# xLSTM block with two feed-forward layers in one kernel: layer one in four chunks of 2, 3, 3 and 4 tiles

## What is computed

```python
for t in range(S):                       # B, H = 2, 8; S = 768; D = 40
    m_new = np.maximum(f_gate[t] + m, i_gate[t])
    f_stab, i_stab = np.exp(f_gate[t] + m - m_new), np.exp(i_gate[t] - m_new)
    C = f_stab * C + i_stab * outer(v[t], k[t]);  n = f_stab * n + i_stab * k[t]
    y[t] = sigmoid(o_gate[t]) * (C @ q[t]) / np.maximum(np.abs(n @ q[t]), 1.0)
x = y.reshape(1536, 320)
xn = x / rms(x) * rms_g                  # layer one, 1536 hidden features
x = (silu(xn @ w_gate) * (xn @ w_val)) @ w_out
h = x @ w_in                             # layer two, 2048 hidden features
out = np.maximum(0.01 * h, h) @ w_out2
```

## Time and profile before

| | |
|---|---|
| runs | 440.17 us median of 3 (439.88 to 440.44) |
| profiled execution | 440.19 us, span 438.5 us |
| TensorE busy | 98% of the span, 3237 matmuls |
| VectorE, ScalarE, POOL busy | 52%, 44%, 21% |
| granted TensorE clock | full throughout |

### The profile page before, as it was taken

The page is one execution under the profiler, slowest core; times in us unless marked ns, Lnnn a source line. Parts: engine busy times, 40 slices in busy tenths (PEclk is TensorE's granted clock), DMA queues, the critical chain, the costliest instruction groups (busy, mean ns, idle before and its releaser), DMA issues.

```text
span 438.5 us, 8229 instructions
## 1 busy us (share of the span) xinstructions
PE 429.8 (98%) x3237; PEld 377.7 (86%) x3237; DVE 226.3 (52%) x439; ACT 193.3 (44%) x428; POOL 91.0 (21%) x97
## 2 busy tenths in 40 slices
PE   7999999999999999999999999999999999999997
PEld 5889999999788888878888888989999999999996
DVE  8856656775466555456433335353333333533534
ACT  4867753665262535235333226553343343333332
POOL 1798852212111111002333004430000000000000
PEclk9999999999999999999999999999999999999999
DMA  7887623431202410001222102300000000100101
GB/s 213 279 294 257 215 86 124 126 121 51 78 27 98 131 47 0 1 1 33 66 67 66 34 1 67 100 0 1 0 1 0 1 1 1 44 17 0 61 0 60
DMA packets 10692, 30.42 MB, mean 69 GB/s; under 512 B 1296, under 2 KB 3264, under 8 KB 10656
## 3 DMA queue, kind: packets, MB, share of 16 engines
q1 hardware_dynamic: 10656, 29.92, 21.4%
HBM read 27.90 MB, written 2.01 MB: 68 GB/s over the span
## 4 chain that ended last, share of the span: by engine, by line
PE 82%; issue 6%; POOL 4%; DMA 4%; DVE 3%; ACT 1%; SPq 0%; POOLq 0%; DVEq 0%
PE gate_ps L1166 22%; PE value_ps L1166 22%; PE out_ps L1243 9%; PE out_ps L1205 9%; PE turn_ps L1243 6%; PE out_ps L1209 3%; PE c_ps L1243 3%; PE turn_ps L1131 3%; POOL w_sb L483 2%; DMA raw<-in_w 2%; PE turn_ps L1092 1%; DMA att_sb<-in_tok 1%; PE turn_ps L1109 1%; PE c_ps L1121 1%; DMA y_acc<-in_first_gates 1%
## 5 line engine op out<-in xcount | busy, mean ns | idle before, releaser
L1166 PE MATMUL value_ps<-x_hi,w_sb 128*128 128x512 f32 (+1 forms) x280 | 68.6, 367 | 0.5 <-DVE h_lo L929 0.5
L1166 PE MATMUL gate_ps<-x_hi,w_sb 128*128 128x512 f32 (+1 forms) x280 | 68.8, 368 | 0.2
L1166 PEld LDWEIGHTS gate_ps<-x_hi,w_sb 128*128 128x128 f32 x280 | 47.4, 191 | 8.2 <-DVE x_odd L895 1.1
L1166 PEld LDWEIGHTS value_ps<-x_hi,w_sb 128*128 128x128 f32 x280 | 47.7, 191 | 7.4 <-DVE h_lo L929 0.7
L908 DVE SCALAR_TENSOR_TENSOR act_buf<-act_buf,gate_ps 128x512 f32<-128x512 f32 (+1 forms) x46 | 26.2, 569 | 48.1 <-ACT act_buf L619 47.9
L934 DVE TENSOR_TENSOR h_lo<-hid,h_hi 128x512 fp32r<-128x512 f32 x48 | 33.2, 692 | 33.7 <-ACT h_hi L638 33.7
L633 ACT ACTIVATE h_hi<-value_ps 128x512 fp32r<-128x512 f32 (+1 forms) x46 | 23.0, 500 | 58.4 <-DVE value_ps L915 58.2
L1205 PE MATMUL out_ps<-h_hi,w_sb 128*128 128x512 f32 (+1 forms) x184 | 48.2, 348 | 0.0
L638 ACT ACTIVATE h_hi<-hid 128x512 fp32r<-128x512 f32 x48 | 30.3, 632 | 37.6 <-DVE hid L922 36.5
L619 ACT ACTIVATE act_buf<-gate_ps 128x512 f32<-128x512 f32 (+1 forms) x46 | 23.1, 501 | 49.3 <-PE gate_ps L1166 49.1
L1243 PE MATMUL out_ps<-w_sb,h_hi 128*128 128x320 f32 x192 | 43.0, 309 | 0.2 <-DVE h_lo L934 0.2
(11 more groups left out here) (148 smaller groups left out, 797.5 us busy)
## 6 DMA issues: line engine op xcount, KB each, us to landing
raw<-in_w SPq DMA_DIRECT2D x12, 544.0 KB, 4.6
att_sb<-in_tok SPq DMA_DIRECT2D x12, 484.0 KB, 4.8
raw<-in_w SPq DMA_DIRECT2D x16, 352.0 KB, 3.0
expo<-decay_scratch SPq DMA_DIRECT2D x10, 512.0 KB, 5.3
att_sb<-in_qk SPq DMA_DIRECT2D x24, 160.0 KB
out_y<-y_acc SPq DMA_DIRECT2D x12, 160.0 KB, 1.9
consts_sb<-in_consts SPq DMA_DIRECT2D x1, 129.5 KB, 2.7
y_acc<-in_first_gates SPq DMA_DIRECT2D x1, 112.0 KB, 2.6
```

Source lines behind the costliest of these rows:

```text
L1166: last = nc.tensor.matmul(ps[:, 0:n], lhs, rhs, start=(j == 0), stop=(j == len(xs) - 1))
```

## The change

Layer one's chunks are tiles 0 and 1; 2 to 4; 5 to 7; 8 to 11, each through all 12 feature tiles: 12 steps of 256 columns, 24 of 384 and 12 of 512, 48 steps. `narrow` (half a slot, out1 two steps behind) holds for the steps of 2 tiles alone. The output banks are now filled from column 0 in every chunk and taken to x for layer two four times. In `BESIDE`, tile 4's R, O and T stand one step earlier and tile 5's S one step later. In POOL's list exponents(5) goes from ahead of fade_state(4) to behind inverse_rms(4).

```diff
--- before.py
+++ after.py
-SPLIT = 10
-STEPS = ([(t0, FIRST, f) for t0 in (0, FIRST) for f in range(SPLIT)]
-         + [(0, CHUNK_TILES, f) for f in range(SPLIT, NF1)]
-         + [(c * CHUNK_TILES, CHUNK_TILES, f) for c in range(1, CHUNKS) for f in range(NF1)])
+CHUNKS1 = [(0, FIRST), (2, 3), (5, 3), (8, 4)]
+STEPS = [(t0, tiles, f) for t0, tiles in CHUNKS1 for f in range(NF1)]
 STEPS1 = len(STEPS)
-LAST1 = [max(s for s, (t0, _, _) in enumerate(STEPS) if t0 < (c + 1) * CHUNK_TILES) for c in range(CHUNKS)]
+LAST1 = [(c + 1) * NF1 - 1 for c in range(len(CHUNKS1))]
-BESIDE = {2: (1, 2, 3, 4), 3: (4, 5, 6, 7), 4: (7, 9, 10, 11), 5: (10, 12, 13, 14), 6: (14, 15, 16, 17),
+BESIDE = {2: (1, 2, 3, 4), 3: (4, 5, 6, 7), 4: (7, 8, 9, 10), 5: (11, 12, 13, 14), 6: (14, 15, 16, 17),
...
         def narrow(s):
-            return s < STEPS1 and STEPS[s][1] * P < CHUNK
+            return s < STEPS1 and STEPS[s][1] == FIRST
...
-        def cols2(c):
-            return slice(c * CHUNK, (c + 1) * CHUNK)
+        def made(c):
+
+            t0, tiles = CHUNKS1[c]
+            return slice(t0 * P, (t0 + tiles) * P), tiles * P
+
+        def chunks_in(c):
+
+            return 1 + min(i for i, (t0, tiles) in enumerate(CHUNKS1) if t0 + tiles >= (c + 1) * CHUNK_TILES)
...
             lo_weights(10)
-            exponents(5)
             fade_state(4)
             lo_weights(11)
             inverse_rms(4)
+            exponents(5)
             weigh_keys(5)
...
             def x2_high(c):
                 act.wait_ge(out_done, after(LAST1[c]))
-                cols, n = cols2(c), CHUNK
+                cols, n = made(c)
...
             def out1(s):
                 pe.wait_ge(h_done, s + 1)
-                t0, tiles, f = STEPS[s]
-                c, t = divmod(t0, CHUNK_TILES)
-
-                cols = slice(t * P, (t + tiles) * P)
+                f = STEPS[s][2]
+                c = s // NF1
+                cols = slice(0, width(s))
...
-                    pe.wait_ge(x2_done, c + 1)
+                    pe.wait_ge(x2_done, chunks_in(c))
```

More of the change, by code:

```diff
@@ L1036, in _ @@
             steps2(STEPS1 + RING, STEPS1 + GF)
-            x2_odd(CHUNKS - 1)
+            x2_odd(len(CHUNKS1) - 1)
             steps2(STEPS1 + GF, STEPS1 + (CHUNKS + 1) * GF)
@@ L1205, in out1 @@
                         nc.tensor.matmul(out_ps[k][:, cols], lhs, rhs[:, r, place],
-                                         start=(f == 0 and t == 0 and j == 0), stop=(f == NF1 - 1 and j == 2))
+                                         start=(f == 0 and j == 0), stop=(f == NF1 - 1 and j == 2))
                 free(2)
@@ L1209, in out1 @@
                     last = nc.tensor.matmul(out_ps[2][:, cols], w[:, W1M:W1M + P], rhs[:, r, place],
-                                            start=(f == 0 and t == 0 and j == 0), stop=(f == NF1 - 1 and j == 1))
+                                            start=(f == 0 and j == 0), stop=(f == NF1 - 1 and j == 1))
                 last.then_inc(out_done, 1)
@@ L1237, in out2 @@
                         if 0 <= out_bank < KT:
-                            pe.wait_ge(x2_taken, KT * (CHUNKS - 1) + out_bank + 1)
+                            pe.wait_ge(x2_taken, KT * (len(CHUNKS1) - 1) + out_bank + 1)
                         before = i * CHUNK_TILES + k - len(y_banks)
```

## The result

The changed kernel takes 443.48 us (median of 6 runs, 442.28 to 443.86), the kernel before 440.31 us (median of 6 taken with it). The ratio is 1.0069, with a 95% interval of 1.006 to 1.0079: slower by 3.2 us or 0.7%. My forecast was 442.2 us and slower. The direction is right; the loss is 1.1 us larger than my sum. The median itself lies 0.08 us above the end of my range, 443.4 us; as a change on the kernel before, +3.17 us, it lies just inside it (+0.7 to +3.2 us on the 440.19 us that I added to), so the range was kept with nothing to spare. The profiled execution took 443.32 us, 3.13 us over that of before.

The account below looks back on a forecast made before the run. TensorE was taken as the bound: its matmuls plus few waits. Matmuls 0.64, waits gone -0.52, -0.54 and -0.60 (tile 4's turn), tile 4 earlier 0.18, chunk start 2.9: +2.06 us on 440.19, forecast 442.2 us, range 440.9 to 443.4.

Parts of the forecast that it names:

- Matmuls, +0.64 us: Steps go from 46 to 48: 48 more TensorE matmuls, each costing a fixed 0.0133 us whatever its width.
- Waits that go, -0.52 and -0.54 us: Gates 24 and 36 no longer wait for x (-0.52); state products of tiles 5, 6, 7 lose 0.18 us each (-0.54).
- Tile 4 a step earlier, +0.18 us: Tile 4's state products, now in iteration 9 one step after tile 3's turn, gain a 0.18 us wait.
- The new start of a chunk, +2.9 us: Gate 12 waits for tile 4's x behind tile 5's exponentials on ScalarE: start at 71.2 instead of 68.3 us.
- rival 4: TensorE idling nearly 3 us is granted 1.2 GHz for a step: up to 446.4 us; chance 0.02.
- the 0.18 us of my list: TensorE waiting around state products when the tile before was turned one narrow step earlier; listed for tiles 5, 6 and 7.
- Rivals 1 and 2: Gate 12's chain partly hidden, wait 1.7 us or less, 441.05 us, chance 0.15; or wholly hidden, 439.35 us, chance 0.05.
- three ScalarE blocks: Argument against a partly hidden chain to gate 12: three ScalarE blocks of 1.2 to 1.3 us in a row cannot shrink.
- Rival 3: Gate 13, value 13 or out1 of step 12 also waits, 1 to 1.5 us: 443.4 us; chance 0.05.

Follow-up runs that it names:

- the three rearrangements: On the changed kernel, singly: exponents(5) ahead of fade_state(4), 441.37 us; out1 of step 10 ahead of gate 12, 440.51; second half of tile 5's exponentials behind x_high, 440.46.
- Filling the stretch: The changed kernel with 16 matmuls of 256 columns that compute nothing of use, placed ahead of gate 12: 441.53 us.
- The rearranged kernels: the three rearrangements; all three together, 439.6 us; the changed kernel with tile 5's S at step 10 and exponents(5) ahead of fade_state(4), 440.29; that plus out1 moved, 439.37.
- both profiles that had one: The changed kernel's first profiled execution, 443.32 us, and the profiled execution of its repeat without any edit, 444.59 us (repeat's median 443.48 us).

## Why the prediction was right and where it was wrong

- **Matmuls, +0.64 us.** 384 columns start 0.174 us apart (forecast 0.173), so the fixed part of 0.0133 us holds at the new width, and 48 more matmuls cost 0.64 us. The isolated gap of the Trainium skill (TensorE: Matmul & The Clock Gate, Back-to-back issue gap) would have 0.1625 us; the trace decides for 0.174.
- **Waits that go, -0.52 and -0.54 us.** Gates 24 and 36 start without a wait; tile 6's state products cost 2.07 us and not 2.24. Both as forecast, the second within 0.1 us over the three tiles.
- **Tile 4 a step earlier, +0.18 us.** Gate 10 is at 61.05 against the 61.1 that holds the term.
- **The new start of a chunk, +2.9 us.** Gate 12 at 71.14 against 71.2, link by link within 0.1 us; the three rearrangements moved it by 0.66, 0 and 1.39 us where 0.65, 0 and 1.45 were expected. Without a wait TensorE would have stood there at 68.4 and not 68.3 (gate 10 at 61.05, two narrow steps of 2.88, the turn 0.41, the scores 1.18), so the term is 2.74 us.
- **What failed is rival 4's weight.** The sum has no term for the clock: it ran TensorE at full clock behind the idle stretch, on the ground that the clock row of before showed full clock everywhere. That row could not speak on it: before had no idle stretch of this length in layer one. (Nor does it show every fall, as the last section says.) Filling the stretch gave 1.5 us back, and 2.06 + 1.5 = 3.6 us against the 3.13 us between the profiles. So the forecast came near, and the range held, because this missing cost was partly made up by what the next point counts: that is luck. I had priced this rival at up to 4.2 us (a whole step at half clock); it cost 1.5 us in one execution and 2.7 us in another.
- **What is left.** With the clock out of it, my sum is too high by about 0.4 us: 3.13 - 1.5 = 1.6 us against 2.06. The rearranged kernels say the same, coming out 0.2 to 0.7 us below what I wrote. The two timelines, laid side by side iteration by iteration, show three pieces of about 0.16 us. One is the term above, 2.74 us in place of 2.9. The others are small costs of the kernel before that I did not list. Tile 8's state products, behind a tile turned only just before, took 2.21 us there (from gate 22 at 115.15 to its value at 119.17, less the gate's 1.81) and take 2.06 us now (126.40 to 129.85, less 1.39): it is the 0.18 us of my list, a fourth time. And the iteration with tile 11's turn and the one behind it (189.02 to 200.67, less two steps of 5.44) cost 0.77 us over their plain steps, and cost 0.35 us now (185.84 to 194.51, less two of 4.16): 0.42 us gone where I had 0.26. The other differences cancel to within 0.1 us, and layer two takes the same time in both. The rows on tile 8, before and then now:

```profile
119.17 1.19 PE L1166 MATMUL value_ps<-x_hi,w_sb 128*128 128x512 f32 x4
```

```profile
126.40 0.85 PE L1171 MATMUL gate_ps<-x_hi,w_sb 128*128 128x384 f32 x4
...
129.85 0.96 PE L1171 MATMUL value_ps<-x_hi,w_sb 128*128 128x384 f32 x4
```

- **Rivals 1 and 2** (part or all of the chain hidden) needed the dates to move, and they did not. Of the "three ScalarE blocks" that I set against rival 1 two are ScalarE's (1.28 and 1.26 us); the third, of 1.10 us, is POOL's affine select. **Rival 3**, a second wait right behind: with the gap filled gate 13 follows value 12 by 3.29 us, which its matmuls alone explain (3.31), so there is none.

The range should have reached to rival 4: the wait that I forecast myself was the condition for it.

## What to carry to other kernels

When work is moved beside other work, follow the queue of every engine that issues it in its program order: here the harm was not on TensorE, whose step had room, but in one tile's exponentials and a copy that came to stand ahead of another tile's x_high on ScalarE. A chain with each link read from the one trace of the kernel before gave the new date to 0.1 us. When such a sum itself yields an idle stretch of TensorE of a few microseconds, price the clock behind it too; and look for work that is already due, here an out1, to put into it.

## What the runs showed of the hardware

An idle stretch of 2.2 us in the midst of dense matmuls brought the granted clock down to 1.2 GHz in both profiles that had one. The shares missing from 1.00 make some 3.4 us at the lower level in the first profile ((0.37 + 0.06) x 4 / 0.5) and 6.9 us in the second ((0.45 + 0.41) x 4 / 0.5), the end of the idle stretch included. With idle rests of 1.5, 1.05, 0.8 and 1.0 us the clock stayed full there in the profiled executions, one each. The Trainium skill, TensorE: Matmul & The Clock Gate, section Why this matters for your kernels, warns of idle gaps between bursts; these runs agree with it. Sixteen matmuls that compute nothing made the kernel 1.5 us faster by the profiles, 1.95 us by the medians.

The clock row's 8 in slice 2 is another low stretch, at the start of layer one (0.67 from 20 to 25 us), and it teaches caution with that row. The kernel before has it too, though its row says 9 there. The end of its first gate, from TensorE's timeline of before:

```profile
21.99 0.63 PE L1166 MATMUL gate_ps<-x_odd,w_sb 128*128 128x256 f32 x2
22.42 1.06 PE L1166 MATMUL value_ps<-x_hi,w_sb 128*128 128x256 f32 x4
```

Matmuls of 256 columns start 0.215 us apart here (two from 21.99 to 22.42) where they start 0.120 us apart later: one column per cycle at 1.2 GHz would be 0.213. So the pace of equal matmuls shows a fall that the granted clock of that trace does not, and a full row by itself is no proof of a full clock. The forecast does not hang on this, since the paces that it used were read at 84 and at 183 us. Both kernels are slow there and gate 9 starts at 55.84 us in both. What brings that fall about is not shown: no idle stretch of 2 us stands right ahead of it.
